# Delta-rule attention and two MoE layers on one core: the first chunk's solve in two halves, its keys-by-queries made ahead

## The reference

```python
k_n = k / (norm(k) + 1e-6)
for t in range(S):                       # S = 768
    y[:, :, t] = q[:, :, t] @ state
    v_old = state.T @ k_n[:, :, t]
    state = state + beta[t] * outer(k_n[:, :, t], v[:, :, t] - v_old)
x = y, tokens by (head, dim)             # 3072 x 384
h = x @ w_in;  g = h if h >= 1, 0 if h <= -1, else (h + 1)**2 / 4;  x = g @ w_out
h = x @ w_in2; r = max(h, 0);            out = (r * r) @ w_out2
```

## Time and profile before

| | us |
|---|---|
| three runs | 1010.06, 1008.83, 1010.09 (median 1010.06) |
| profiled execution | 1011.17 |
| its span | 1009.4 |
| TensorE matmul busy | 987.5 (98%) |
| VectorE busy | 589.4 (58%) |
| ScalarE busy | 415.8 (41%) |
| GpSimd busy | 10.3 (1%) |

### The profile page before, as it was taken

One profiled execution on the slowest core, in us unless ns is written; L12 is line 12 of the kernel. 1 busy time (PEld: TensorE's weight loads), 2 busy tenths in 40 slices (PEclk: granted clock), 3 DMA queues, 4 the chain that ended last, 5 costly groups with the idle time before them and its releaser, 6 DMA issues.

```text
span 1009.4 us, 24269 instructions
## 1 busy us (share of the span) xinstructions
PE 987.5 (98%) x10460; PEld 806.8 (80%) x10460; DVE 589.4 (58%) x1113; ACT 415.8 (41%) x737; POOL 10.3 (1%) x21
## 2 busy tenths in 40 slices
PE   4999999999999999999999999999999999999998
PEld 3677788888888888888888888888888888888887
DVE  6868987876877686768644774333433333334332
ACT  4548543434443344434434554323333333323333
POOL 2000000000000000000000000000000000000000
PEclk7969999999999999999999999999999999999999
DMA  7133133003200320021002521001010010000000
GB/s 265 51 99 106 41 93 92 34 17 90 86 10 19 93 76 9 18 58 47 2 4 84 197 73 63 1 1 63 1 62 1 1 63 1 6 26 1 32 0 32
DMA packets 28409, 50.93 MB, mean 50 GB/s; under 512 B 2320, under 2 KB 15760, under 8 KB 28304
## 3 DMA queue, kind: packets, MB, share of 16 engines
q1 hardware_dynamic: 28304, 49.39, 15.3%
HBM read 39.94 MB, written 9.44 MB: 49 GB/s over the span
## 4 chain that ended last, share of the span: by engine, by line
PE 95%; DVE 2%; ACT 1%; issue 1%; DMA 0%; DVEq 0%; ACTq 0%
PE psum L1025 39%; PE psum L1001 38%; PE psum L832 3%; PE psum L874 2%; PE psum L810 2%; PE psum L846 2%; PE psum L855 1%; PE psum L788 1%; PE psum L915 1%; PE psum L907 1%; PE psum L953 1%; PE psum L902 1%; PE psum L939 1%; PE psum L930 1%; PE psum L771 1%
## 5 line engine op out<-in xcount | busy, mean ns | idle before, releaser
L1025 PE MATMUL psum<-g_hi,w 128*128 128x512 f32 x1152 | 392.0, 395 | 0.0
L1001 PE MATMUL psum<-x_hi,w 128*128 128x512 f32 x1152 | 386.7, 390 | 0.2 <-DVE x_lo L1237 0.2
L1025 PEld LDWEIGHTS psum<-g_hi,w 128*128 128x128 f32 x1152 | 216.2, 188 | 50.6 <-issue 2.0
L1255 DVE TENSOR_TENSOR g_lo<-act_g,g_hi 128x512 fp32r<-128x512 f32 x192 | 132.5, 690 | 211.2 <-ACT g_hi L679 211.2
L1001 PEld LDWEIGHTS psum<-x_hi,w 128*128 128x128 f32 x1152 | 216.2, 188 | 46.4 <-issue 1.0
L679 ACT ACTIVATE g_hi<-act_g 128x512 fp32r<-128x512 f32 x192 | 121.4, 632 | 273.8 <-PE psum L1025 239.2
L1025 PE MATMUL psum<-g_lo,w 128*128 128x512 f32 x576 | 224.6, 390 | 0.0
L1001 PE MATMUL psum<-x_lo,w 128*128 128x512 f32 x576 | 224.2, 389 | 0.0
L1249 DVE TENSOR_TENSOR act_g<-act_g 128x512 f32<-128x512 f32 x96 | 66.4, 691 | 112.9 <-ACT act_g L672 112.9
L1001 PEld LDWEIGHTS psum<-x_lo,w 128*128 128x128 f32 x576 | 108.1, 188 | 22.1
L1025 PEld LDWEIGHTS psum<-g_lo,w 128*128 128x128 f32 x576 | 108.2, 188 | 20.6
(11 more groups left out here) (96 smaller groups left out, 601.8 us busy)
## 6 DMA issues: line engine op xcount, KB each, us to landing
kt_sb<-in_k_t SPq DMA_DIRECT2D x24, 256.0 KB, 4.1
qt_sb<-in_q_t SPq DMA_DIRECT2D x24, 256.0 KB, 3.5
kn_sb<-in_k_n SPq DMA_DIRECT2D x20, 256.0 KB, 4.1
ring<-in_v_s SPq DMA_DIRECT2D x24, 192.0 KB, 2.9
between_layers<-y_out SPq DMA_DIRECT2D x6, 768.0 KB, 3.7
x_sb<-between_layers SPq DMA_DIRECT2D x6, 768.0 KB, 5.7
result<-y_out SPq DMA_DIRECT2D x5, 768.0 KB, 4.2
wi_st<-in_w_in SPq DMA_DIRECT2D x7, 384.0 KB, 3.2
```

Of the source, the lines that this page charges most:

```text
L1001: ins = pe.matmul(h_ps[n % 2][:, :], w_in_part(layer, f // GW, part)[:, kt, fs], x[:, kt, :], start=(kt == 0 and j == 0), stop=(kt == KT - ...
L1025: ins = pe.matmul(acc[kt][:, :], w_out_part(layer, f // GW, part)[:, f % GW, ds], g[n % 2][:, :], start=(f == 0 and j == 0), stop=(f == NF ...
L1255: dve.tensor_tensor(g_lo[n % 2][:, :], act_g[n % 2][:, :], g_hi[n % 2][:, :].bitcast(F32), ALU.subtract).then_inc(g_lo_ready, 1)
```

## The change

It touches chunk 0 and what stands ahead of it, and the form of the inverse in all chunks.

- *Solve in halves.* The four row blocks of chunk 0 are solved for heads 0 to 3 and 4 to 7 apart, in two PSUM banks (`first_solve`, `first_substitute`, `residual_first`, `solved_first`). Of the four copies per half ScalarE makes three (`OWN = 3`) and VectorE one.
- *Keys by queries ahead.* All four items of chunk 0 are multiplied before the low parts, copied by ScalarE as they are (`kq_out`), and masked in place by GpSimd with `affine_select` once `xc` is ready.
- *Inverse.* Each step's outer product and addition are done for even rows and odd rows in turn, four operations for two; `tmp` has room for both.
- *Gains.* The maximum with 1e-30 becomes a bias in the root, factors 0.5 and -1 are folded in; the turn of the norms moves behind `start_inverse` in chunk 0.
- *TensorE's start.* Three products of zeros ahead of the Gram blocks; fewer `keep_busy` products ahead of the solve, now in bank 0.
- *ScalarE's order.* Two Gram copies, root, two Gram copies, chunk 1's diagonals, keys by queries, then the weight splits, low parts and scaling; the split of group 2 and the scaling of block 3 move ahead of and into the solve.
- *Outputs.* Their high and low parts are made from PSUM, item by item (`x_high_first`, `x_low_first`), without `x1`.
- *Loads.* Queries go ahead of the values; both weight groups, values 1 to 3, the last queries and the next groups each wait for an earlier load; values 4 to 7 and all behind them wait for chunk 0's outputs.

```diff
+            pool.wait_ge(xc_ready, 1)
+            for m in range(B):
+                for hp in range(2):
+                    pool.wait_ge(kq_plain, 2 * m + hp + 1)
+                    pool.affine_select(out=kq_of(m, hp), in_=kq_of(m, hp), compare_op=ALU.is_gt, fill=0.0, base=0,
+                                       pattern=[[0, HP], [1, P]], channel_multiplier=-1).then_inc(kq_ready, 1)
...
             for b in range(B):
                 first_diagonals(b)
+            act.wait_ge(gd0_ready, NB * B)
+            gram_out(0)
+            gram_out(1)
             gain_root(0)
+            gram_out(2)
+            gram_out(3)
+            gd_out(1, 0)
+            gd_out(1, 1)
             for m in range(B):
-                gram_out(m)
+                kq_out(m)
             split_weights(0, 0, 0)
             split_weights(0, 0, 1)
-            gd_out(1, 0)
             split_weights(0, 1, 0)
             split_weights(0, 1, 1)
-            gd_out(1, 1)
             low_out(0, 0)
             low_out(0, 1)
-            scaled_first(0)
+            scaled_first(0, 0, H)
             low_out(1, 0)
             low_out(1, 1)
-            for k in range(1, NB):
-                scaled_first(k)
-            for k in range(NB):
-                for b in range(3 if k == 0 else 2):
-                    solved(k, b)
-                if k == 0:
-                    gain_root(1)
+            scaled_first(1, 0, H)
+            scaled_first(2, 0, H)
             split_weights(0, 2, 0)
             split_weights(0, 2, 1)
+            for k in range(NB):
+                for part in range(HALVES):
+                    for b in range(OWN):
+                        solved_first(k, part, b)
+                    if k < 2:
+                        scaled_first(NB - 1, 2 * (HALVES * k + part), 2 * (HALVES * k + part) + 2)
+                if k == 1:
+                    gain_root(1)
             for m in range(B):
-                x_out(m)
-            x_high(0, 0)
+                x_high_first(m)
             gram_out(B)
...
+            pe.wait_ge(tmp_zero, 1)
+            for _ in range(3):
+                pe.matmul(bank[7][:, 0:2 * P], tmp[:, 0:P], tmp[:, 0:2 * P], start=True, stop=True)
             for b in range(B):
                 first_grams_of(b)
             for hp in range(2):
                 diagonals_of(1, hp)
+            for m in range(B):
+                keys_by_queries(m)
...
-            for j in range(23, BLK - 1):
-                pe.wait_ge(inv_chain, 2 * j + 2)
-                keep_busy((3 if j < 27 else 2) * P, bank[4])
+            for j in range(26, BLK - 1):
+                pe.wait_ge(inv_chain, inv_count(j))
+                keep_busy(2 * P, bank[0])
             pe.wait_ge(inv_chain, CH)
-            keep_busy(4 * P, bank[4])
-            keep_busy(3 * P, bank[4])
-            for k in range(NB):
-                solve(k)
-                keys_by_queries(k)
-                if k < NB - 1:
-                    substitute(k + 1)
-                    keep_busy(2 * P, bank[4])
+            keep_busy(4 * P, bank[0])
+            keep_busy(2 * P, bank[0])
+            for part in range(HALVES):
+                first_solve(0, part)
+            for k in range(1, NB):
+                keep_busy(2 * P, bank[0])
+                for part in range(HALVES):
+                    first_substitute(k, part)
+                for part in range(HALVES):
+                    first_solve(k, part)
+            keep_busy(2 * P, bank[0])
...
-                    outer = tmp[:, 0:(j + 1) * w].rearrange("p (r c) -> p r c", r=j + 1)
-                    chain(n, 2 * j + 2)
-                    dve.tensor_tensor(outer, diag[:, j:j + 1, j + 1:BLK].to_broadcast(part),
-                                      x_inv[:, 0:j + 1, j:j + 1].to_broadcast(part), ALU.mult).then_inc(inv_chain, 1)
-                    chain(n, 2 * j + 3)
-                    dve.tensor_tensor(x_inv[:, 0:j + 1, j + 1:BLK], x_inv[:, 0:j + 1, j + 1:BLK], outer,
-                                      ALU.add).then_inc(inv_chain, 1)
+                    for odd, count, _ in rows:
+                        part = [P, count, w]
+                        chain(n, at - 1 + odd if j > 1 else at)
+                        dve.tensor_tensor(outer[odd], diag[:, j:j + 1, j + 1:BLK].to_broadcast(part),
+                                          x_inv[:, odd:j + 1:2, j:j + 1].to_broadcast(part), ALU.mult).then_inc(inv_chain, 1)
+                    for odd, count, _ in rows:
+                        chain(n, at + 1 + odd)
+                        dve.tensor_tensor(x_inv[:, odd:j + 1:2, j + 1:BLK], x_inv[:, odd:j + 1:2, j + 1:BLK], outer[odd],
+                                          ALU.add).then_inc(inv_chain, 1)
...
-            load_v(0)
             for m in range(B, 2 * B):
                 load_kt(m)
+            for m in range(QUERIES):
+                load_qt(m)
+            load_v(0)
+            sp.wait_ge(kt_loaded[KEYS - 1], 16)
             load_weights(0, 0, w_in1, w_out1)
+            sp.wait_ge(v_loaded[0], 16)
             load_weights(0, 1, w_in1, w_out1)
+            sp.wait_ge(ws_loaded[0], 32)
             for k in range(1, RING):
                 load_v(k)
-            for m in range(QUERIES):
-                load_qt(m)
-            load_weights(0, EARLY, w_in1, w_out1)
+            sp.wait_ge(ws_loaded[1], 32)
+            load_qt(B - 1)
             for m in range(2):
                 load_kn(m)
+            sp.wait_ge(qt_loaded[0], 32)
+            load_weights(0, EARLY, w_in1, w_out1)
             load_weights(0, 2, w_in1, w_out1)
-            load_qt(B - 1)
+            sp.wait_ge(y_done, B)
```

More of the change, by code:

```diff
@@ L45 @@
 STEP = BLK + 1
+EVEN_PART = max((j + 2) // 2 * (BLK - 1 - j) for j in range(BLK))
+ODD_PART = max((j + 1) // 2 * (BLK - 1 - j) for j in range(BLK))
+HALVES = 2
+HH = H // HALVES
+OWN = 3
 def wait(eng, sem, value):
@@ L278, in block_rows, with half_heads, half_pairs @@
             return slice(i * BLK, (i + 1) * BLK)
+        def half_heads(part):
+            return slice(part * HH, (part + 1) * HH)
+        def half_pairs(b, part):
+            return slice(b * HP + part * HP // 2, b * HP + (part + 1) * HP // 2)
         def u_of(head, rows):
@@ L856, in substitute, with first_substitute, first_solve @@
                                             gram[b][0:i * BLK, place(0, j), (i - 1) * BLK:i * BLK],
[L857 removed]
+                                            u_of(b * H + j, i * BLK), start=False, stop=(j == H - 1))
                             if j == H - 1:
                                 ins.then_inc(s_done, 1)
+            def first_substitute(k, part):
+                before = HALVES * (k - 1) + part + 1
+                pe.wait_ge(first_u_act, OWN * before)
+                pe.wait_ge(first_u_dve, (B - OWN) * before)
+                pe.wait_ge(gram_ready, 2 * B)
+                for j in range(part * HH, (part + 1) * HH):
+                    for b in range(B):
+                        at = j % HH * D
+                        ins = pe.matmul(chain_ps[part][block_rows(b), at:at + D],
+                                        gram[b][0:k * BLK, place(0, j), (k - 1) * BLK:k * BLK],
+                                        u_of(b * H + j, k * BLK), start=True, stop=True)
+                ins.then_inc(first_s_done, 1)
+            def first_solve(k, part):
+                if k:
+                    pe.wait_ge(first_r_ready, HALVES * (k - 1) + part + 1)
+                else:
+                    pe.wait_ge(kq_plain, 2 * (B - 1))
+                pe.wait_ge(scaled0, H * k + (part + 1) * HH)
+                pe.wait_ge(xc_ready, 1)
+                for j in range(part * HH, (part + 1) * HH):
+                    for b in range(B):
+                        rows, at = block_rows(b), j % HH * D
+                        ins = pe.matmul(chain_ps[part][rows, at:at + D], xc[rows, place(k, j), :], ring[rows, k, j, :],
+                                        start=True, stop=True)
+                ins.then_inc(first_t_done, 1)
             def solve(k):
                 n, i = divmod(k, NB)
[L864 to L869 removed]
+                pe.wait_ge(r_ready, k - NB + 1)
                 pe.wait_ge(xc_ready, n + 1)
@@ L1110, in chain, with diagonal @@
                 wait(dve, inv_chain, CH * n + k)
-            def diagonal(n):
+            def diagonal(n, first=0, past=BLK):
                 if n:
@@ L1210, in ahead @@
                     diagonal(n)
-                if at == 1:
-                    gains(n, half_of)
+                if at == 1 and not half_of:
+                    gains_norm(n)
+                if at == 1 and half_of:
+                    gains_square(n)
+                    gains_value(n)
+                    gains_turn(n)
                 if at == 2 and not half_of:
```

308 lines of the change are left out of this document (183 added, 125 removed).

## The result

Ten runs of the changed kernel have a median of 1006.38 us (1005.52 to 1008.10), ten of the kernel before 1009.88 (1007.27 to 1012.88). The ratio is 0.9967, 95% interval 0.9955 to 0.9980: 3.3 us faster, 2.0 to 4.5. Forecast were 7.0 us, 1003.1. The time lies inside the stated range (999.5 to 1008.0) and the sign was right, but the gain is less than half of the one forecast.

The account below looks back on a forecast made before the run. A fixed 938 us TensorE block leaves only the 71.32 us ahead, with ScalarE's line late; 1.4 (ScalarE earlier) + 5.25 (chain) + 0.15 = 6.8, taken as 7.0 with a shrinking wait: 1010.06 - 7.0 = 1003.1 us, range 999.5 to 1008.0.

Parts of the forecast that it names:

- 43.5 (42.2 to 46.0): Start of ScalarE's first solved copy in us, with bounds, summed as 24.7 + 13.4 + 3.7 + 1.7; before it was 44.95.
- Products of zeros, 1.4 us won: Ahead of the Gram blocks: full pace comes 2.8 us earlier, so the grams end at 8.5 instead of 9.93 us.
- 1.3 us of the 3.75: TensorE's instruction stop amid chunk 1's diagonals, 3.75 us before: 1.3 us of it taken, as the loads ahead are thinner.
- land at 19.1: Queries of the fourth keys-by-queries item, held behind both weight groups, land at 19.1 us, not later than their turn.
- Low parts as before, 13.4: From the low parts' start to the end of the last low part: 13.4 us, as before the change.
- rival 3: ScalarE's line is earlier, no stop and full clock through diagonals and low parts: first copy 41.0, time 1000.6; chance 0.10.
- Gains 0.5 and inverse 2.4: VectorE's line in chunk 0: gains 0.5 us shorter, inverse 2.4 us shorter at 0.08 us in each of 30 steps.
- rival 4: Inverse gets slower: VectorE operations do not overlap, it takes 11.4 us more, xc at 52.0, time 1016.7; chance 0.06.
- Copies of 0.33 us, rounds of 4.2, chain 14.4: Four blocks: ScalarE's halved copies 0.33 us, rounds 4.2, first copy to outputs 14.4 instead of 19.65.
- Rival 2: Halved solved copies in the chain cost the full 0.48 us: 3.6 us more, time 1006.7; chance 0.12.
- Outputs to first product, 0.15 won: Outputs' start to first product: 0.6 us added for the clock, 0.75 won by parts straight from PSUM, net 0.15.
- Rival 1: ScalarE's line is later: whole 3.75 us stop stays, clock at half, first copy 46.0, time 1005.6; chance 0.13.

Follow-up runs that it names:

- run 2: The changed kernel with the inverse as before, one outer product and one addition per step over all rows: 1007.29 us, 0.9959 of the kernel before.
- run 5: The changed kernel with weight group 2's two splits on ScalarE put back behind the chain of four blocks: 1005.16 us, 0.9952 of the kernel before.
- run 8: The changed kernel with earlier splits, VectorE scaling blocks 1 to 3, group 2's splits later, copies two and two, no keep-busy ahead of the solve: 999.74 us, 0.9896.
- run 1: The changed kernel without the three products of zeros ahead of the Gram blocks: 1006.00 us, 0.9951 of the kernel before.
- run 6: The changed kernel with values of blocks 1 to 3 scaled by VectorE instead of by 24 small ScalarE operations: 1004.55 us, 0.9946 of the kernel before.
- run 11: The changed kernel with the first weight groups and all loads behind them held until chunk 1's diagonals are done: 1010.90 us, one run.
- run 3: The kernel before with only the inverse by even and odd rows: 1010.21 us, 0.9991 of the kernel before.
- run 9: The kernel of run 7 with chunk 0 solved whole instead of in halves: 1007.56 us, 0.9974 of the kernel before.
- run 10: The changed kernel with loads in the order of before and not held back, only the fourth queries ahead of weight group 2: 1008.21 us, 0.9978.
- run 7: The changed kernel with solved copies shared two and two between ScalarE and VectorE instead of three and one: 1004.38 us, 0.9942 of the kernel before.

## Why the prediction was wrong

The view was right: a block of 938 us that nothing changes, and ScalarE with TensorE ahead of the solve as the late line. Run 2 shows it, and runs 5 and 8 show it by moving that line. The step that failed is the time of the first solved copy, "43.5 (42.2 to 46.0)"; it was 48.29. Its terms, each as predicted and as measured in the changed kernel:

| term of that sum | predicted | measured |
|---|---|---|
| start of chunk 1's diagonals | 10.35 | 13.24 |
| diagonals, with the stop | 4.1 + 1.3 | 6.5, stop 2.98 |
| from their end to the low parts | 9.0 | 9.0 |
| low parts to the last copy | 13.4 | 14.6 |
| to the first solved copy | 5.4 | 5.0 |

- *Products of zeros, 1.4 us won.* Wrong: the Gram blocks ended 1.2 us later in this profile. I read one rise of the clock as a fixed delay from the start of work; run 1 and the spread over the profiles show that it varies from one execution to the next. In the sum this term is 2.7 of the 4.8 us. It would not have come through whole: in run 6, with the same program up to there, the Gram blocks ended at 9.06, 2.1 us earlier, the stop was 3.70, and the last low part's copy ended only 0.9 us earlier (42.42 for 43.32).
- *The stop, "1.3 us of the 3.75".* Measured 2.98. Run 11 gives a floor that I didn't have: 1.64 even with DMA idle. The value was below anything that the runs show.
- *The fourth item's queries, which "land at 19.1".* Wrong: `load_qt` waits for item 0's products, which free the buffer, so they were issued at 21.88, and TensorE waited 0.54 us for them at 25.47 (1.67 in run 2). The 9.0 us of this stretch came out right all the same, by luck.
- *Low parts as before, 13.4.* 1.2 us more: I had seen the 2.7 us of idling ahead of them, and used it only as an argument against rival 3, not as a price for my own sum. That the idling is the cause is not shown: in run 1 the low parts took 13.3 us after the same idling, because full clock was back 3.5 us after their start instead of 6.0.
- *Gains 0.5 and inverse 2.4.* Measured 0.7 (14.24 to 16.42, before 2.86) and 2.95 (17.78 to 38.18, before 23.35). A step at 256 elements takes 0.81 (27.55 to 28.36) where 0.92 stood. Operations in a pair start 0.08 to 0.1 before the other's end, with semaphore waits on all of them, and rival 4 fell. The rule of the Trainium skill that the prediction cited (VectorE: DVE Perf Modes, "The DRAIN you can't avoid") does not hold for such a pair; the prediction left out that the same section lets a next operation that is not held start earlier, which is what the trace shows. That all of it is hidden was right (runs 2 and 3).
- *Copies of 0.33 us, rounds of 4.2, chain 14.4.* Right: copies 0.99 for three, rounds 3.5, 4.5 and 3.8, chain 13.84 (13.8 to 14.7 over the eight profiles with three copies). Rival 2 fell: a copy of 192 elements takes 0.33, not 0.48. That the halves themselves carry it is shown by run 9 (3.2 us, a part of it the clock's); that keys by queries and masks left the chain was not tried by itself.
- *Masks by GpSimd, 1.16 us each.* Measured 0.60 (3.57 for six), done by 45.1. Hidden, as said.
- *Outputs to first product, 0.15 won.* Measured 1.68. I had kept the clock at half there; it came back at 58.7, ahead of the outputs. Not all of it is the clock: in run 9, where full clock was back only 1.5 us into the outputs, the stretch took 5.73 us, 1 us less than before. This error went the other way and covered 1.5 us of the first, which is luck.
- *Loads held back cost nothing.* Right that nothing behind the first product waits for them. Whether holding them back won time ahead of it is open (run 10: 1.1 us by the ratios, inside the intervals).

Together: first copy +4.8, chain -0.6, outputs -1.5 make 2.7 us of the 2.9 by which the span's gain (4.1) fell short of 7.0. The timed gain is 0.8 us smaller still (3.3), which is within its interval. The size of the miss at the first copy is not the luck of one execution: it stands at 48.2 to 48.4 in four profiles with this order ahead of it (the changed kernel, runs 2, 7 and 9), and run 1's, without the products of zeros, lies at 45.84, just inside the predicted 42.2 to 46.0. Rival 1, a later line of ScalarE, had the right mechanism, 0.13 of the chance and too small a price (2.5 us).

## What to carry to other kernels

When two lines meet at one point, shortening the one that is already early is worth nothing, and every item moved ahead of the meeting on the other (here copies, splits, scalings and filler products) is paid in full: count the queue of each engine there, fillers too. Then even the load between them: giving 24 small scalings and a second copy of each half to VectorE, splits an earlier place and the solve a free TensorE brought 7 us more than the change. What stands beside the path in the rounds (8 of these scalings) cost nothing. And where a clock's rise or a fetch stands in a sum, take it as a range over several executions, not from the one profile at hand.

## What the runs showed of the hardware

- The first record of full clock on TensorE stood between 4.7 and 10.9 us over eleven profiles in which it starts dense work at 1.25 us. VectorE's line moves with it: xc was ready at 37.3 to 38.8 us where that record stood at 6.5 us or earlier, and at 39.8 to 40.3 where it stood at 10 or later, with the same inverse.
- TensorE's stream stopped for its own instructions 1.64 us with idle DMA (one execution) and 2.3 to 3.75 us with DMA full, and went on 1.2 to 1.6 us after a 16 KB packet of the instruction queue had ended.
- GpSimd's select of 128x512 takes 0.60 us, twice the one of 128x128 for four times the elements.
- On VectorE 31 steps of an outer product and an addition took 23.35 us as dependent pairs and 20.40 us as interleaved even and odd rows, with nearly twice as many operations.
